# Expert kernel after linear attention: a second tile picked ahead, weight splits moved to GpSimd, attention's end and the first tiles reordered

## The chip, the cores and the metric

One Trainium2 chip, one core of it. The metric is the device time of one execution in microseconds (us). The engines are TensorE (PE, matmuls; PEld is its weight load), VectorE (DVE), ScalarE (ACT), GpSimd (POOL) and SyncE (SP), which in this kernel only issues DMAs.

## The reference

Three stages. First attention with a fading state, for 4 batches, 8 heads, 768 steps, 48 channels:

```
state = f[t] * state + k[t] (outer) v[t];   y[t] = q[t] @ state
```

Its output, 3072 tokens of 384 columns, goes to a layer of 8 experts. Each token takes the expert with the largest `x @ w_gate + bias[modality]`; `h = relu(x @ w1[e])` (1024 wide), `out = prob * (h @ w2[e])`. Last comes a gated layer on all tokens: a norm, `silu(xn @ w_gate) * (xn @ w_val)` (1536 wide), `@ w_out`. All in float32.

## The kernel before, in words

**Precision.** A float32 product is made from three matmuls: every operand is split in a rounded part (hi) and the rest (lo), and hi hi + lo hi + hi lo is summed (`three`, L1777). So each weight and each activation costs a rounding copy on ACT (hi) and a subtraction on DVE (lo).

**Attention** (`attention`, from L245) runs over CH = 6 chunks of 128 steps by B = 4 batches: 24 groups. The five engines each run a `step(c, b, half, more)` in a software pipeline; `tile(c, b, back)` gives the group that is `back` steps behind. In step n PE turns the keys of group n-1 (`ks_ps`), makes its scores, makes the output rows and gate logits of group n-3, and the state growth and the read (`yT_ps`) of group n-2. After the last chunk come four more steps with c = 6. Each finished chunk is routed on DVE: `Routing.choose` finds each token's expert, PE counts (`count`), `Routing.place` gives each token a row in its expert's region of `x_regions` in memory; GpSimd scatters the rows there (L137, four scatters per chunk). At c = 6 the chunk routed is the fifth. The sixth is chosen, counted, placed and scattered in the expert stage.

**Picked ahead.** `Ahead.pick` (L191 on) runs on DVE after four chunks: the expert with most tokens so far has a full tile of 256 tokens already, and SP loads its weights (`load_weights`) and rows (`load_rows`) while attention ends. ACT and DVE split w1 and x in the last four steps (`hi_w1`, `lo_w1`, `hi_x`, `lo_x`); w2 is split in the first tile.

**Barriers.** A block of engine programs ends with a barrier of all five engines. Then each reads a flag that says whether the fast attention was exact enough (`general_attention`, not run here), and a second barrier follows.

**Experts** (`experts`, from L1104). Tiles of 256 tokens of one expert, 13 of them here, in order j = 0 to 12 by `tiles` (L1263): `body(0, "first")`, a loop of `"middle"` ones, and `"last"`. On PE (`body` at L1801) a tile is: hidden(0), hidden(1), gather_y(0), hidden(2), gather_y(1), hidden(3), the turn of the next tile's x, gather_y(2), gather_y(3). hidden(g) is 18 matmuls into `h_ps`, gather_y(g) 12 into `y_ps`. In the first tile the count of the last chunk stands between hidden(0) and hidden(1) and waits for choose (`marks`, 7). gather_y(g) waits for `h_split` (DVE's lo_h, L1691) and `w2_split` (DVE's lo_w2, L1664).

ACT and DVE have their own written-out order for each place: hi_h(g) (L1484) and lo_h(g), next_w1(g) and next_w2(g) for the next tile's weights (L1457, L1461 and L1658, L1664), hi_x and lo_x. In the first tile DVE also computes `table_of_tiles` (which expert and which rows each tile has), `shifted_scores`, `rows_of_tiles`, and at its end `rows_of_tokens` and `gates_of_tokens`.

SP issues, in order, the loads of w1, x, w2 (one buffer each, so a piece is loaded when the piece of the tile before is split), the stores of y, a block of padding rows (`pad`), and the six thirds of the last stage's weights (`load_third`, into `g_in`), and its output weights at tile 7 (`WO_AT`). All of SP's loads for tile 1 wait for `table_ready`. ACT rounds thirds 0 and 1 in the first tile and one each at the end of tiles 1 to 4; GpSimd makes their lo part (L1419, three subtractions of 128x512 each) and, after each third, four scatters of gates (`by_token`, L1422).

The last stage (`body2`) is not touched but for the first square and the table load.

## Time and profile before

| | us |
|---|---|
| median of 3 runs | 866.95 (866.81 to 869.07) |
| the profiled execution | 866.84 |
| its span (first to last instruction) | 865.1 |
| TensorE busy in the span | 833.0 (96%), 5332 matmuls |
| DVE busy | 471.8 (55%), 773 instructions |
| ACT busy | 389.6 (45%) |
| GpSimd busy | 165.6 (19%) |
| mean granted TensorE clock | 0.988 |

The chain of work that ended last is 78% TensorE. Attention lies at 0 to 157.7, the experts at 160.3 to about 407, the gated layer behind them. In the page's list the clock is 9 or more tenths in nearly all of the 40 slices. Times in the rows are counted from the start of the span. `[3.17 <-issue]` at the end of a row means that the engine was idle for 3.17 us before this instruction, and what the profile names as releaser.

### The profile page before, as it was taken

What the parts mean: (1) busy time and instruction counts of PE and PEld (TensorE: products, weight loads), DVE (VectorE), ACT (ScalarE), POOL (GpSimd) and SP (SyncE); (2) the same over time, 40 slices, a digit from 0 to 9 for tenths busy, and PEclk for the clock granted to TensorE, in tenths of its full rate; (3) what the DMA queues carried; (4) which work ended last, traced back from release to release, by engine and by line L of the source; (5) the groups of instructions that cost most, each with busy time, mean ns of one, the idle gap of its engine ahead of it and who ended that gap; (6) DMA issues with size and microseconds to landing.
All of it is one profiled execution on the core that took longest, in us unless ns stands there. A gap on an engine that the chain in (4) does not pass through costs nothing.

```text
span 865.1 us, 15457 instructions
## 1 busy us (share of the span) xinstructions
PE 833.0 (96%) x5332; PEld 762.5 (88%) x5332; DVE 471.8 (55%) x773; ACT 389.6 (45%) x750; POOL 165.6 (19%) x165
## 2 busy tenths in 40 slices
PE   6999999779999999989999999999999999999997
PEld 6798988779999999989888888888888898888887
DVE  7989898687766666653444333334333333433332
ACT  5988786375666555653423411331241133123112
POOL 5444352318554000000000200100020010001001
PEclk9999999889999999999999999999999999999999
DMA  9877666497988797750200200100020000000000
GB/s 182 188 148 169 150 146 210 153 387 239 301 258 260 245 344 255 255 147 20 74 1 1 74 0 1 66 8 0 0 73 0 0 28 8 0 0 36 0 0 36
DMA packets 44082, 96.49 MB, mean 112 GB/s; under 512 B 9168, under 2 KB 25040, under 8 KB 43920
## 3 DMA queue, kind: packets, MB, share of 16 engines
q1 hardware_dynamic: 39952, 85.81, 33.6%
q0 software_dynamic: 3840, 9.47, 3.1%
q10 hardware_dynamic: 256, 0.79, 0.4%
q8 instruction: 18, 0.29, 0.1%
q14 instruction: 16, 0.13, 0.1%
HBM read 76.75 MB, written 19.29 MB: 111 GB/s over the span
## 4 chain that ended last, share of the span: by engine, by line
PE 78%; issue 2%; DVE 1%; POOL 0%; ACT 0%; DVEq 0%; ACTq 0%
PE h_ps L1779 16%; PE h_ps L1781 15%; PE h_ps L1780 15%; PE ym_ps L1779 7%; PE ym_ps L1781 7%; PE ym_ps L1780 7%; PE xTm_ps L1780 3%; PE xTm_ps L1779 3%; PE xTm_ps L1781 3%; PE xT_ps L1796 1%; PE xTm_ps L1787 1%; POOL out L1443 0%; DVE h_lo L1691 0%; DVE w_lo L1664 0%; ACT w_hi L1461 0%
## 5 line engine op out<-in xcount | busy, mean ns | idle before, releaser
L1754 DVE TENSOR_TENSOR gs<-h_ps,sig 128x512 f32<-128x512 f32 x72 | 49.8, 691 | 175.5 <-ACT sig L1555 175.5
L1555 ACT ACTIVATE sig<-h_ps 128x512 f32<-128x512 f32 x72 | 43.1, 598 | 158.9 <-PE h_ps L1781 158.9
L1566 ACT CAST h_hi<-hid 128x512 fp32r<-128x512 f32 x72 | 44.6, 620 | 150.2 <-DVE hid L1757 150.2
L1779 PE MATMUL h_ps<-x_hi,w_hi 128*128 128x256 f32 x312 | 89.7, 287 | 7.7 <-DVEq L1682 5.1
L1781 PE MATMUL h_ps<-x_lo,w_hi 128*128 128x256 f32 x312 | 89.3, 286 | 0.0
L1780 PE MATMUL h_ps<-x_hi,w_lo 128*128 128x256 f32 x312 | 89.1, 285 | 0.0
L1779 PE MATMUL h_ps<-w_hi,wg_hi 128*128 128x512 f32 x216 | 85.5, 396 | 0.0
L1781 PE MATMUL h_ps<-w_lo,wg_hi 128*128 128x512 f32 x216 | 84.6, 392 | 0.0
L1781 PE MATMUL h_ps<-w_lo,wv_hi 128*128 128x512 f32 x216 | 84.2, 390 | 0.0
L1780 PE MATMUL h_ps<-w_hi,wv_lo 128*128 128x512 f32 x216 | 84.0, 389 | 0.0
L1779 PE MATMUL h_ps<-w_hi,wv_hi 128*128 128x512 f32 x216 | 84.0, 389 | 0.0
L1780 PE MATMUL h_ps<-w_hi,wg_lo 128*128 128x512 f32 x216 | 83.9, 388 | 0.0
L1757 DVE TENSOR_TENSOR hid<-h_ps,gs 128x512 f32<-128x512 f32 x72 | 49.8, 692 | 57.5 <-PE h_ps L1781 57.5
L1779 PE MATMUL ym_ps<-w_hi,h_hi 128*128 128x384 f32 x208 | 73.0, 351 | 7.1 <-issue 3.5
L1664 DVE TENSOR_TENSOR w_lo<-w_in,w_hi 128x768 fp32r<-128x768 f32 x52 | 55.1, 1061 | 36.2 <-ACT w_hi L1461 36.1
L1767 DVE TENSOR_TENSOR h_lo<-hid,h_hi 128x512 fp32r<-128x512 f32 x72 | 49.8, 692 | 44.7 <-ACT h_hi L1566 44.7
L1781 PE MATMUL ym_ps<-w_lo,h_hi 128*128 128x384 f32 x208 | 71.2, 342 | 0.0
L1780 PE MATMUL ym_ps<-w_hi,h_lo 128*128 128x384 f32 x208 | 71.0, 342 | 0.0
L1779 PEld LDWEIGHTS h_ps<-x_hi,w_hi 128*128 128x128 f32 x312 | 60.7, 194 | 8.4 <-DVEq L1682 5.2
L1780 PEld LDWEIGHTS h_ps<-x_hi,w_lo 128*128 128x128 f32 x312 | 60.4, 194 | 0.0
L1781 PEld LDWEIGHTS h_ps<-x_lo,w_hi 128*128 128x128 f32 x312 | 60.4, 194 | 0.0
L1461 ACT CAST w_hi<-w_in 128x768 fp32r<-128x768 f32 x52 | 43.3, 835 | 34.2 <-PE ym_ps L1781 27.5
(222 smaller groups left out, 1890.0 us busy)
## 6 DMA issues: line engine op xcount, KB each, us to landing
w_raw<-in_w SPq DMA_DIRECT2D x52, 384.0 KB, 5.0
w_in<-in_w SPq DMA_DIRECT2D x52, 384.0 KB, 5.1
qkf_in<-in_qkf SPq DMA_DIRECT2D x43, 288.0 KB, 5.0
y_sorted<-x_group SPq DMA_DIRECT2D x13, 384.0 KB, 3.4
v_in<-in_v SPq DMA_DIRECT2D x24, 192.0 KB, 4.3
x_regions<-zero_row SPq DMA_DIRECT2D x12, 384.0 KB, 2.9
x_group<-x_regions SPq DMA_DIRECT2D x12, 384.0 KB, 3.9
g_in<-in_wg SPq DMA_DIRECT2D x3, 768.0 KB, 8.1
```

Of the source, the lines that this page charges most:

```text
L1461: nc.scalar.copy(w2_hi[:, 2 * g:2 * g + 2].rearrange("p b d -> p (b d)"), w2_in[:, g]).then_inc(w2_hi_done, 1)
L1555: nc.scalar.activation(sig[:], g_ps, ACT.Sigmoid).then_inc(sig_done, 1)
L1566: nc.scalar.copy(h2_hi[:, fb % HELD], hid[:]).then_inc(h2_hi_done, 1)
L1664: nc.vector.tensor_tensor(w2_lo[:, 2 * g:2 * g + 2].rearrange("p b d -> p (b d)"), w2_in[:, g], w2_hi[:, 2 * g:2 * g + 2].rearrange("p b d ...
L1754: nc.vector.tensor_tensor(gs[:], g_ps, sig[:], ALU.mult).then_inc(gs_done, 1)
L1757: nc.vector.tensor_tensor(hid[:], v_ps, gs[:], ALU.mult).then_inc(hid_done, 1)
L1767: nc.vector.tensor_tensor(h2_lo[:, fb % HELD], hid[:], h2_hi[:, fb % HELD].bitcast(F32), ALU.subtract).then_inc(h2_split, 1)
L1779: nc.tensor.matmul(out, hi, rhs_hi, start=first, stop=False)
L1780: nc.tensor.matmul(out, lo, rhs_hi, start=False, stop=False)
L1781: return nc.tensor.matmul(out, hi, rhs_lo, start=False, stop=last)
L1787: mm = nc.tensor.transpose(xT_ps[:, k, s * P:(s + 1) * P], x_in[:, s, k * P:(k + 1) * P], ident[:])
L1796: mm = nc.tensor.transpose(xT2_ps[:, k % 2, q * P:(q + 1) * P], y_in[par][:, q, k * P:(k + 1) * P], ident[:])
```

## The change

It has these parts.

1. **Attention's end.** The key turns and the copy `ks` of the last group are left out (nobody reads them). PE's read of a group is now a function `read`, and that of the last group goes into `ks_ps` right after the one before it, ahead of the output rows of group 22. ACT's order of rounding copies changes; the split of w1's fourth piece on DVE (`lo_w1(3)`) moves behind the barriers. SP issues the eight weight loads ahead of the last two v loads.
2. **A second pick.** `pick_next`, 12 small DVE instructions at the start of the expert stage, finds the expert with most tokens left after five chunks and the row from which its tile starts. SP loads tile 1's weights and x from it at once, and not from the table. `table_of_tiles` and `rows_of_tokens` allow for two tiles out of order.
3. **w2 of the first tile.** ACT rounds all four pieces before hi_h(0), GpSimd subtracts (four times 128x768), ahead of the last chunk's scatters, and signals on `made`.
4. **New order in the first tiles.** DVE: pick_next, choose, lo_w1(3), lo_h(0), place, lo_h(1), table, and so on. `rows_of_tiles` goes to the first tile's end, `shifted_scores`, `rows_of_tokens` and `gates_of_tokens` to the ends of tiles 1, 2 and 3. The thirds are rounded at the ends of tiles 1 to 6, the gates' scatters stand behind thirds 3 to 5 (eight each), output weights are loaded at tile 8. The exp is in tile 2.
5. **Last tile.** ACT takes hi_h(0) before the squares, and loads its table of functions there.

```diff
@@ class Ahead
+    def pick_next(self, nc, rt, link, ready):
+        link(nc.vector.tensor_tensor(self.has[:], rt.base[:], self.start[:], ALU.subtract))
+        link(nc.vector.tensor_reduce(self.most[:], self.has[:], AX.X, ALU.max))
+        link(nc.vector.tensor_scalar(self.has[:], self.has[:], self.most[:, 0:1], None, ALU.is_equal))
+        link(nc.vector.tensor_tensor(self.has[:], self.has[:], rt.rank_e[:], ALU.mult))
+        link(nc.vector.tensor_reduce(self.next_rank[:], self.has[:], AX.X, ALU.max))
+        nc.vector.tensor_scalar(self.next_f[:], self.next_rank[:], -1.0, float(E), ALU.mult, ALU.add)
+        nc.vector.tensor_scalar(self.next_expert[:], self.next_rank[:], -1.0, float(E), ALU.mult, ALU.add)
+        link(nc.vector.tensor_scalar(self.next_one[:], rt.rank_e[:], self.next_rank[:, 0:1], None, ALU.is_equal))
+        link(nc.vector.tensor_tensor(self.next_at[:], self.next_one[:], self.start[:], ALU.mult))
+        nc.vector.scalar_tensor_tensor(self.start[:], self.next_one[:], float(TM), self.start[:], ALU.mult, ALU.add)
+        link(nc.vector.tensor_reduce(self.next_row_f[:], self.next_at[:], AX.X, ALU.add))
+        nc.vector.tensor_scalar(self.next_row[:], self.next_row_f[:], 1.0, None, ALU.add).then_inc(ready, 1)
@@ attention, sync
-            for b in range(2):
-                load_v(*tile(CH, b, 2))
             sp.wait_ge(ahead_sems.picked, PICKS)
             e = first.expert_of(sp)
             first.load_weights(sp, e, w1, w2, ahead_sems)
+            for b in range(2):
+                load_v(*tile(CH, b, 2))
@@ attention, scalar
+                if at(c, CH) and b == 1:
+                    first.hi_w1(nc, act, 3, ahead_sems)
+                    kept(tile(c, b, 2), ks_ps)
...
-                if at(c, CH) and b < 2:
-                    first.hi_w1(nc, act, 2 * b, ahead_sems)
...
                 if at(c, CH) and b == 0:
-                    first.hi_w1(nc, act, 1, ahead_sems)
+                    for g in range(2):
+                        first.hi_w1(nc, act, g, ahead_sems)
+                if (t := tile(c, b, 2)) and not (at(c, CH) and b == 1):
+                    kept(t, yT_ps)
+                if at(c, CH) and b == 0:
+                    first.hi_w1(nc, act, 2, ahead_sems)
@@ attention, vector
-                if at(c, CH) and b == 2:
+                if at(c, CH) and b == 1:
+                    first.lo_w1(nc, dve, 2, ahead_sems)
                     dve.wait_ge(flag_sum, 1)
...
+                if at(c, CH) and b == 2:
+                    first.lo_x(nc, dve, xT_ps, ahead_sems)
                 if t := tile(c, b, 3):
...
-                if at(c, CH) and b == 2:
-                    first.lo_x(nc, dve, xT_ps, ahead_sems)
-                    first.lo_w1(nc, dve, 3, ahead_sems)
@@ attention, tensor
                     pe.wait_ge(scaled, n + 1)
-                    wait_past(pe, ks_done, n)
-                    for j in range(PR):
-                        mm = nc.tensor.transpose(ks_ps[:, j], kT[:, s, j], ident[:])
-                    mm.then_inc(k_turned, 1)
+                    if not at(c, CH):
+                        wait_past(pe, ks_done, n)
+                        for j in range(PR):
+                            mm = nc.tensor.transpose(ks_ps[:, j], kT[:, s, j], ident[:])
+                        mm.then_inc(k_turned, 1)
...
+                if at(c, CH) and b == 1:
+                    pe.wait_ge(ks_done, NT - 1)
+                    read(c, b, tile(c, b, 2), ks_ps)
+                    pe.wait_ge(small_ready, 1)
+                    nc.tensor.matmul(flag_ps, rt.ones_r[:], small[:], start=True, stop=True).then_inc(flag_sum, 1)
                 if t := tile(c, b, 3):
@@ experts, sync
-            for i in range(EARLY):
-                load_third(i)
-            sp.dma_start(norm.g_norm[:], rms_g).then_inc(norm_in, 16)
...
                 if place == "first":
                     sp.wait_ge(table_ready, 1)
-                    e1 = expert(1)
-                    pad(e1)
+                    e1 = sp.value_load(first.next_expert[0:1, 0:1], min_val=0, max_val=E - 1)
+                    row = sp.value_load(first.next_row[0:1, 0:1], min_val=0, max_val=E * REGION - TM)
                     for g in range(GR):
                         sp.wait_ge(w1_split, g + 1)
                         load_w1(e1, g)
+                    sp.dma_start(x_in, x_regions[bass.ds(row, TM), :].rearrange("(s p) d -> p s d", p=P)).then_inc(x_landed, 16)
+                    for g in range(GR):
+                        sp.wait_ge(made, MADE + g + 1)
+                        load_w2(e1, g)
+                    for i in range(EARLY + 1):
+                        load_third(i)
                     sp.wait_ge(scattered, 16 * B)
-                    load_x(1)
-                    for g in range(GR):
-                        sp.wait_ge(w2_split, g + 1)
-                        load_w2(e1, g)
-                    load_third(EARLY)
-                    sp.wait_ge(rows_ready, 1)
+                    sp.wait_ge(table_ready, 2)
@@ experts, gpsimd
+            for g in range(GR):
+                pool.wait_ge(w2_hi_done, g + 1)
+                nc.gpsimd.tensor_tensor(w2_lo[:, 2 * g:2 * g + 2].rearrange("p b d -> p (b d)"), w2_in[:, g],
+                                        w2_hi[:, 2 * g:2 * g + 2].rearrange("p b d -> p (b d)").bitcast(F32), ALU.subtract
+                                        ).then_inc(made, 1)
             pool.wait_ge(marks, Routing.PLACED)
@@ experts, scalar
-            hi_w2(0, 0)
+            for g in range(GR):
+                hi_w2(0, g)
...
+                hi_h(0)
+                if place != "first":
+                    next_w1(0)
                 if place == "last":
                     act.wait_ge(norm_in, 16)
                     square(0, 0)
-                hi_h(0)
+                hi_h(1)
+                if place == "last":
+                    nc.scalar.preload_act_table_set("sigmoid_and_others")
@@ experts, vector
+            first.pick_next(nc, rt, link, table_ready)
             rt.choose(nc, dve, CH - 1, marks, 0)
-            lo_w2(0, 0)
-            dve.wait_ge(counted, 1)
-            rt.place(nc, dve, CH - 1, LAST_HALF, pre_ps, cnt_ps, marks, 0)
+            lo_w1(0, GR - 1)
...
                 lo_h(0)
                 if place == "first":
-                    table_of_tiles()
+                    dve.wait_ge(counted, 1)
+                    rt.place(nc, dve, CH - 1, LAST_HALF, pre_ps, cnt_ps, marks, 0)
...
                 lo_h(1)
+                if place == "first":
+                    table_of_tiles()
...
                 if place == "first":
-                    rows_of_tokens()
-                    gates_of_tokens()
+                    rows_of_tiles()
+                if place == "middle":
+                    with dve.If(j < 4):
+                        with only(dve, j, 1):
+                            shifted_scores()
+                        with only(dve, j, 2):
+                            rows_of_tokens()
+                        with only(dve, j, 3):
+                            gates_of_tokens()
@@ experts, tensor
-                    pe.wait_ge(w2_split, j * GR + g + 1)
+                    if place == "first":
+                        pe.wait_ge(made, MADE + g + 1)
+                    else:
+                        pe.wait_ge(w2_split, j * GR + g + 1)
```

## Rows read from the trace of the kernel before

**Rows 1.** Busy time per stretch: length, engines busy (instructions), TensorE clock, DMA share, GB/s.
```profile
155.30:160.30 5.00, 0.00 (x1) 0.03 (x1) 2.04 (x4) 1.19 (x2) 0.79 (x5) 0.81 0.18 66
...
160.30:184.80 24.50, 22.42 (x130) 21.79 (x130) 19.12 (x58) 13.96 (x19) 4.40 (x7) 0.83 0.78 279
...
184.80:209.20 24.40, 19.74 (x127) 19.23 (x127) 19.40 (x29) 12.21 (x18) 16.07 (x13) 0.93 0.89 316
...
209.20:226.90 17.70, 17.70 (x128) 17.68 (x127) 14.12 (x14) 11.56 (x16) 11.33 (x9) 1.00 0.87 275
...
192.50:196.20 3.70, 3.65 (x12) 3.68 (x13) 2.80 (x3) 0.00 (x0) 3.70 (x3) 0.54 1.00 386
...
178.90:182.60 3.70, 3.70 (x16) 3.61 (x16) 3.52 (x6) 2.62 (x4) 0.00 (x0) 0.55 1.05 413
```

**Rows 2.** Timeline of TensorE: start, length; in brackets the idle time before.
```profile
160.30 0.55 PE L1779 MATMUL h_ps<-x_hi,w_hi 128*128 128x256 f32 x1 [5.06 <-DVEq L1682]
...
178.28 0.44 PE L1779 MATMUL ym_ps<-w_hi,h_hi 128*128 128x384 f32 x1 [1.83 <-DVE h_lo L1691]
...
192.55 0.66 PE L1779 MATMUL ym_ps<-w_hi,h_hi 128*128 128x384 f32 x1 [3.17 <-issue]
...
207.05 0.44 PE L1779 MATMUL ym_ps<-w_hi,h_hi 128*128 128x384 f32 x1 [1.49 <-DVE h_lo L1691]
...
393.43 0.42 PE L1779 MATMUL ym_ps<-w_hi,h_hi 128*128 128x384 f32 x1 [0.32 <-issue]
```

**Rows 3.** Attention's end: last scatter, DVE's last subtraction, GpSimd's last wait.
```profile
154.80 0.97 POOL L137 DMA_INDIRECT x_regions<-x_group,row  x1 [0.30 <-issue]
...
156.76 0.95 DVE L226 TENSOR_TENSOR w_lo<-w_raw,w_hi 128x768 fp32r<-128x768 f32 x1
...
L516 POOLq EVENT_SEMAPHORE  x1: 43/43/43, 157.4 to 157.4; - x1
```

**Rows 4.** Timeline: DVE's bookkeeping and its place in an ordinary tile.
```profile
172.51 0.36 DVE L1623 TENSOR_TENSOR scratch<-scratch,most_all 128x192 f32<-128x192 f32 x1
...
187.56 0.16 DVE L1636 SCALAR_TENSOR_TENSOR moved_up<-one_expert,tokens_before 128x8 f32<-128x8 f32 x1
...
190.04 0.18 DVE L1648 TENSOR_SCALAR pos<-pos_f 128x24 uint32<-128x24 f32 x1
...
190.72 0.30 DVE L1654 RECIPROCAL of_token<-total 128x24 f32<-128x24 f32 x1
...
191.76 0.69 DVE L1691 SCALAR_TENSOR_TENSOR h_lo<-h_ps,h_hi 128x512 fp32r<-128x512 f32 x1 [0.73 <-issue]
...
228.40 0.96 DVE L1664 TENSOR_TENSOR w_lo<-w_in,w_hi 128x768 fp32r<-128x768 f32 x1 [1.50 <-ACT w_hi L1461]
...
231.28 0.34 PE L1779 MATMUL ym_ps<-w_hi,h_hi 128*128 128x384 f32 x1
```

**Rows 5.** Timeline: DVE and GpSimd (POOL) side by side, three places.
```profile
201.56 4.84 DVE L1664 TENSOR_TENSOR w_lo<-w_in,w_hi 128x768 fp32r<-128x768 f32 x1 [0.64 <-ACT w_hi L1461]
...
201.78 3.79 POOL L1419 TENSOR_TENSOR wg_lo<-g_in,wg_hi 128x512 fp32r<-128x512 f32 x3
...
229.83 5.24 POOL L1419 TENSOR_TENSOR wv_lo<-g_in,wv_hi 128x512 fp32r<-128x512 f32 x3 [7.89 <-ACT wv_hi L1453]
...
232.83 1.09 DVE L1658 TENSOR_TENSOR w_lo<-w_raw,w_hi 128x768 fp32r<-128x768 f32 x1
...
128.94 0.73 DVE L204 TENSOR_SCALAR one_expert<-rank_e,has_rank 128x8 f32<-128x8 f32 x1
...
128.64 1.06 POOL L137 DMA_INDIRECT x_regions<-x_group,row  x1 [8.69 <-DVE row L132]
```

**Rows 6.** Timeline: first and seventh step of choose, ACT's rounding of output weights.
```profile
160.18 0.19 DVE L100 TENSOR_TENSOR biased<-logits,token_bias 128x32 f32<-128x32 f32 x1 [2.47 <-PEq L796]
...
161.56 0.23 DVE L109 TENSOR_TENSOR_SCAN upto<-restart,chosen 128x32 f32<-128x32 f32 x1
...
162.28 0.83 ACT L1461 CAST w_hi<-w_in 128x768 fp32r<-128x768 f32 x1 [5.79 <-SPq L1337]
```

More of the change, by code:

```diff
@@ L544, in step @@
                         neg_logs(*t)
-                if t := tile(c, b, 1):
+                if (t := tile(c, b, 1)) and not at(c, CH):
                     _, s, n = t
@@ L722, in growth, with read @@
                 mm.then_inc(ds_done, 1)
+            def read(c, b, t, acc):
+                cc, s, n = t
+                if not tile(c, b, 1):
+                    pe.wait_ge(masked, n + 1)
+                if at(c, 0):
+                    pe.wait_ge(consts, CONSTS)
+                pe.wait_ge(v_landed[s], (cc + 1) * 16)
+                if not at(c, CH) and not (at(c, 0) and b == 2):
+                    growth(s, n)
+                wait_past(pe, state_done, n - 3)
+                if not at(cc, 0):
+                    for j in range(PR):
+                        nc.tensor.matmul(acc[:, j], state[:, s, j], qT[:, s, j], start=(j == 0), stop=False,
+                                         skip_group_check=True)
+                if at(cc, 0):
+                    pe.wait_ge(yT_zero, 1)
+                for j in range(PR):
+                    for par in range(2):
+                        h, r = 2 * j + par, PAD * par
+                        mm = nc.tensor.matmul(acc[r:r + D, j], v_in[:, s, D * h:D * (h + 1)],
+                                              scores[:, s % 2, par, j], start=at(cc, 0), stop=(at(cc, 0) or j == PR - 1),
+                                              skip_group_check=True)
+                mm.then_inc(y_done, 1)
             def step(c, b, half, more):
@@ L782, in step @@
                 if at(c, CH) and b == 1:
-                    pe.wait_ge(small_ready, 1)
-                    nc.tensor.matmul(flag_ps, rt.ones_r[:], small[:], start=True, stop=True).then_inc(flag_sum, 1)
                     first.turn(nc, pe, xT_ps, ident, ahead_sems)
```

163 lines of the change are left out of this document (70 added, 93 removed).

## The prediction

> **What bounds the kernel now.** I read the stage table first. The ordinary expert tile (209.2 to 226.9) is 17.7 us long and the matmul unit is busy for all of it, at full clock, so nothing that the change does to an ordinary tile can shorten it. Tile 0 takes 24.5 us and tile 1 takes 24.4, with 22.4 and 19.7 us of busy time, and the clock was 0.83 and 0.93 in them [rows 1]. So there are some 13.5 us above the ordinary length in those two tiles, and 5.0 us more in which the matmul unit does nothing between attention and tile 0. That is all the change can win.
>
> The timeline of TensorE then shows where they lie [rows 2]: 5.06 us before the first expert matmul, 1.83 us before group 2's output matmuls of tile 0, 3.17 us in tile 1 before its first output matmul, 1.49 us later in tile 1, 0.32 us in the last tile. After 1.83 and after 3.17 us of idleness the granted clock fell from 2.4 to about 1.2 GHz for a stretch (0.55 and 0.54 over 3.7 us [rows 1]); in 3.7 us at 0.54 the unit does 2.0 us of full-speed work, so each such stretch costs 1.7 us. After 1.49 us it didn't fall.
>
> The DVE, GpSimd and queue rows say who is late. At the end of attention GpSimd waits until 157.4 for its last row scatter to land, and DVE's last subtraction ends at 157.7 [rows 3]; the barrier follows them at once, and then the flag is read by all five engines, 2.3 us that stay. In tile 1 the 3.17 us are DVE's: it works through the rows and gates of the tokens from 187.56 to 191.0 and comes to h_lo only at 191.76 [rows 4]. The 1.49 us come from a DVE subtraction that took 4.84 us instead of 0.96 while GpSimd ran three subtractions of its own [rows 5].
>
> **The change, part by part.** The sum is made against the profiled execution, 866.84 us (span 865.1), 0.11 under the median of the runs.
>
> *Attention's end.* Group 23's key transposes and their copy go (their state is never used), its scores come 0.6 us earlier, and its read goes into the freed buffer, so it needn't wait for the copy of group 22. DVE loses one 768-column subtraction ahead of the barrier (it moves behind it) and does the x subtraction sooner: its end comes some 2.6 us earlier. GpSimd's four scatters however start when DVE has placed the fifth chunk's tokens, which moves by 0.6 us only, and their landing then is at 156.8. The barrier was at 157.7, so the gain is **-0.9** (bounds: -0.5 if the scatters don't move with it, -2.6 if they land early enough not to matter). On SP, the eight weight loads pass two v loads that waited; v is wanted at 147 and lands by about 141, so this is nothing either way.
>
> *Tile 0, DVE.* Ahead of the body DVE now runs pick_next (12 small instructions), then choose, then one 0.96 us subtraction. The matmul unit counts the chosen tokens between hidden(0) and hidden(1), and for that waits for choose. Choose's first and seventh instruction started 1.38 us apart, 0.23 for each with its wait [rows 6]; its whole chain is 1.7, and pick_next at the same price, with some that don't wait, 2.4. Without interference choose ends 4.1 us after DVE starts, at about 163.3, when hidden(0) at half clock also ends: a wait of 0 to 0.8.
>
> *Tile 0, GpSimd.* The four subtractions of the output weights go from DVE to GpSimd, where 128x512 takes 1.26 (three in 3.79 [rows 5]), so 128x768 about 1.9, four of them 7.6 us. ACT's rounding (0.83 each [rows 6]) feeds them from 160.0, so they fill 160.1 to about 168. gather_y(0) to (3) want them at 166, 171, 175 and 178 at the earliest: ready in time. That takes away the 0.25 and 1.83 us stalls and the slow stretch behind them, **-3.9**. But the same 8 us hold all of choose. Two rows show what DVE does beside a subtracting GpSimd: with both operands in SBUF it waited 3.9 us, through all three GpSimd instructions; in another tile it waited 0.13 us for the one running and went first at the next boundary [rows 5]. A DVE instruction on 8 columns took 0.73 us while GpSimd issued a scatter [rows 5], so small ones wait as well. I take one wait per GpSimd subtraction, the milder row: after seven instructions of pick_next (until 160.5) four waits are due (the one-hot compare, the row product, the start update, choose's first sum), the last of them ends at about 167.6, and the other six steps of choose end at 169.1. The wait of the matmul unit is then 169.1 - 163.3 = **+5.8**, and hidden(1) runs part of its 18 matmuls at 1.2 GHz, +1.0; the earlier start of the tile and its count give 0.7 back. Tile 0: -3.9 + 5.8 + 0.3 = **+2.2**, ending at 186.1 instead of 184.8. Lower bound: no waits, -4.7; upper: held through the whole run, +3.3.
>
> The Trainium skill, page "SBUF — State Buffer", section "Who interferes with whom", has a rule that speaks against this part: a DVE instruction with two SBUF inputs and a GpSimd instruction that reads SBUF share one read port, and whichever comes second is blocked until the first has ended. By that rule alone the 0 waits are ruled out and the sum is the forecast's; the row of 4.84 us is worse than the rule, as there DVE lost three turns in a row.
>
> *Tile 1's inputs.* Picked ahead, its weights are loaded from about 168 even in the blocked case, and x behind them; they are wanted from 173 on. ACT and DVE have its splits done before tile 0 ends. The scatters of the last group land at about 179 and hold up only SP's loads for tile 2, wanted at 187 and later. Cost 0. The early loads of g_in move behind them; their first use is now at the end of tile 1.
>
> *DVE's bookkeeping moves.* At tile 0's end only rows_of_tiles is left (1.3 us) in place of 3.5: with 0.7 us of loop entry DVE reaches h_lo about 1.0 us late, so 3.17 becomes 1.0, the slow stretch (1.7) goes, and so does the 1.49, since GpSimd has no subtractions in tile 1: 1.0 - 3.17 - 1.7 - 1.49 = **-5.4**.
>
> In an ordinary tile DVE's last weight subtraction frees it at 229.27, and h_lo, 0.69 long, has to be done by 231.28 [rows 4]: 1.3 us are free. shifted_scores (three of about 0.36 [rows 4], 1.1 in a chain) fits at the end of tile 1, or waits once for the first piece of the g_in subtraction that GpSimd starts at that moment: **+0.3** (0 to 0.7). rows_of_tokens at the end of tile 2 doesn't fit. It had 11 instructions in 2.6 us (187.56 to 190.13) and has 20, the added ones mostly on 1 to 24 columns: 3.8 us. With some 0.5 of loop h_lo starts at 2.3 + 3.8 + 0.5 = 6.6 after the tile's end and ends at 7.4 instead of 4.3: a stall of 3.1. GpSimd runs its three subtractions over the same time; about half of the DVE instructions from there on read two SBUF tensors, and it would be 5.5 if it waited for each of the three. I take **+3.7**, and with a stall of over 3 us a slow stretch, **+1.7** (0 to 1.7). gates_of_tokens at tile 3's end is 1.0: it fits.
>
> *Last tile.* ACT rounds h before it squares, so the 0.32 us go: **-0.3**. The table load, 1.3 us, moves there from tile 0; ACT waits for matmuls for 4 us next, which covers it.
>
> Sum: -0.9 + 2.2 - 5.4 + 0.3 + 3.7 + 1.7 - 0.3 = +1.3, so **868.1 us**. The measurement can tell about 0.3%, 2.6 us, from no change.
>
> **Rivals.** *Small DVE instructions slip between* GpSimd's subtractions in tile 0, and choose ends at 163.3 to 164. Tile 0 then is -4.7 in place of +2.2, and the total 866.84 + 1.3 - 6.9 = **861.2** (858.5 with no slow stretch and a bare 3.1 us stall in tile 3, 863.0 with 5.5). For it: no row shows a small two-tensor DVE instruction beside a subtracting GpSimd, and one of 0.2 us leaves the port soon. Against: the waits of [rows 5].
>
> *DVE is held through whole runs of GpSimd subtractions*, as in the row of 4.84. It decides from the point at which DVE's request comes in the middle of a GpSimd instruction that has others right behind it. Choose ends 1.1 later; shifted_scores waits until 3.3 us after its place, +2.6 over my term; rows_of_tokens +1.8: 868.1 + 5.5 = **873.6**, slower.
>
> *The change doesn't do what it says*: the second pick has under 256 tokens and a 14th tile appears, +17.6. The inputs' counts (about 1000 tokens left for the expert picked) are against it: 1 in 100.
>
> **How the numbers follow.** Forecast 0.45, own range 865 to 871 (the terms' bounds without tile 0's), rival one 0.37, rival two 0.14, the rest on either side 0.04. Of the forecast's 0.45 about 0.06 is faster by over 2.6, 0.24 within, 0.15 slower. Faster: 0.37 x 0.97 + 0.06 = 0.42; same: 0.24 + 0.02 = 0.26; slower: 0.32. The range of 8 in 10 runs from 859.0 to 872.5.
>
> **What would show it.** A gap of TensorE behind hidden(0) of tile 0, and DVE instructions on 8 to 32 columns of 1 us and more beside GpSimd's w_lo: forecast, over 5 us; rival one, under 1. No gap before gather_y(2) of tile 0. Under 1.2 us before tile 1's first output matmul. A gap of 3 to 6 us before tile 3's. If that last gap isn't there, my count of DVE's free time is wrong, and the whole forecast with it.

## The result and the profile after

The changed kernel takes 888.15 us (median of 4 runs, 885.16 to 888.68), the kernel before 868.01 (4 runs, 866.81 to 873.08). The ratio is 1.0214, 95% interval 1.0165 to 1.0262: slower by 2.1%, outside the range of 859.0 to 872.5. The profiled execution took 887.66 us, its span is 885.9, the granted clock 0.976 (before: 865.1 and 0.988).

The timeline of TensorE in the changed kernel, with the idle time in brackets as in [rows 2]:

```profile
161.23 0.55 PE L1823 MATMUL h_ps<-x_hi,w_hi 128*128 128x256 f32 x1 [5.67 <-DVEq L1729]
...
170.61 0.60 PE L117 MATMUL xTm_ps<-upto,before 128*128 128x8 f32 x2 [5.20 <-DVE upto L109]
...
195.26 0.41 PE L1823 MATMUL ym_ps<-w_hi,h_hi 128*128 128x384 f32 x1 [1.12 <-issue]
...
213.95 0.41 PE L1823 MATMUL ym_ps<-w_hi,h_hi 128*128 128x384 f32 x1 [0.71 <-issue]
...
237.54 0.66 PE L1823 MATMUL ym_ps<-w_hi,h_hi 128*128 128x384 f32 x1 [5.61 <-issue]
...
295.95 0.41 PE L1823 MATMUL ym_ps<-w_hi,h_hi 128*128 128x384 f32 x1 [2.19 <-issue]
...
311.04 0.44 PE L1823 MATMUL ym_ps<-w_hi,h_hi 128*128 128x384 f32 x1 [2.02 <-issue]
```

The 1.83, 3.17 and 1.49 us of [rows 2] are gone; 5.20 in tile 0, 1.12 in tile 1 and 5.61 in tile 3 are the gaps that the prediction named. The two at 295.95 and 311.04 it did not. Gone too are the gap before gather_y(2) of tile 0 and the 0.32 us of the last tile. So all four signs that the prediction named came true, and the time was still 20 us off: they looked at tiles 0 to 3 only.

The same by stretches, cut at the turns of x, with two short ones behind tile 0's gap at the end (columns as in [rows 1]):

```profile
161.20:186.80 25.60, 20.37 (x113) 20.07 (x114) 20.92 (x57) 8.92 (x13) 11.55 (x12) 0.69 0.68 249
186.80:203.90 17.10, 15.98 (x116) 15.65 (x115) 11.43 (x20) 9.39 (x14) 0.00 (x0) 1.00 0.87 320
203.90:222.60 18.70, 17.99 (x129) 17.81 (x128) 13.92 (x16) 11.56 (x16) 4.62 (x3) 1.00 0.75 246
222.60:248.10 25.50, 19.89 (x129) 19.71 (x128) 16.95 (x33) 11.81 (x17) 3.74 (x3) 0.87 0.73 226
248.10:265.80 17.70, 17.70 (x128) 17.70 (x127) 12.60 (x16) 11.57 (x16) 5.27 (x3) 1.00 0.73 222
...
283.60:306.10 22.50, 19.87 (x128) 19.35 (x127) 10.66 (x12) 10.58 (x16) 15.09 (x13) 0.92 0.76 209
306.10:326.20 20.10, 18.08 (x129) 17.74 (x128) 13.08 (x14) 12.24 (x17) 13.22 (x10) 1.00 0.66 199
326.20:344.60 18.40, 17.99 (x129) 17.81 (x128) 11.12 (x13) 10.20 (x15) 5.50 (x6) 1.00 0.99 289
...
170.60:175.00 4.40, 4.39 (x20) 4.39 (x21) 2.46 (x10) 0.00 (x0) 1.28 (x2) 0.50 0.98 374
170.60:177.00 6.40, 6.39 (x27) 6.39 (x28) 3.12 (x12) 1.29 (x2) 2.94 (x3) 0.50 1.02 357
```

With the starts of the turns (L1831 here, L1787 before) the two traces are laid side by side. A stretch from one turn to the next is called by the tile whose turn ends it. From the first expert matmul to the turn in tile 0: 25.56 us against 21.52. Then 17.08 against 20.84 (tile 1), 18.69 against 19.48 (tile 2), 25.50 against 17.64 (tile 3), 17.75 and 17.74 (tiles 4 and 5), and 22.54, 20.10, 18.39 (tiles 6, 7 and 8), all against 17.64; every one after them is 17.74 against 17.64. The texts written ahead of the experiments call the three late stretches tiles 5 to 7. From the last turn to the end it is 488.1 us against 484.2. So of the 20.8 us of span, 0.9 lie ahead of the first expert matmul, -0.5 in the three stretches to tile 2's turn, +7.9 in tile 3's, +8.1 in the three of tiles 6 to 8, 0.5 in the ordinary tiles, 3.9 behind the last turn.

DVE and GpSimd in tile 0, where the prediction put its four waits:

```profile
162.27 0.15 DVE L222 TENSOR_SCALAR next_f<-next_rank 128x1 f32<-128x1 f32 x1
...
162.40 1.44 DVE L224 TENSOR_SCALAR next_one<-rank_e,next_rank 128x8 f32<-128x8 f32 x1
163.87 1.74 DVE L225 TENSOR_TENSOR next_at<-next_one,start_behind 128x8 f32<-128x8 f32 x1
165.64 1.72 DVE L226 SCALAR_TENSOR_TENSOR start_behind<-next_one,start_behind 128x8 f32<-128x8 f32 x1
...
167.54 1.61 DVE L100 TENSOR_TENSOR biased<-logits,token_bias 128x32 f32<-128x32 f32 x1
...
170.33 0.23 DVE L109 TENSOR_TENSOR_SCAN upto<-restart,chosen 128x32 f32<-128x32 f32 x1
...
161.97 1.84 POOL L1446 TENSOR_TENSOR w_lo<-w_in,w_hi 128x768 fp32r<-128x768 f32 x1 [0.26 <-ACT w_hi L1506]
```

Each of the four long ones (L224, L225, L226, L100) waits for one GpSimd subtraction, and none for two. The instruction on one column at 162.27 did not wait, though GpSimd's subtraction had begun at 161.97. In tile 3, DVE's rows of the tokens and GpSimd's three subtractions:

```profile
230.96 0.69 DVE L1683 TENSOR_SCALAR in_first<-row_all,first_row 128x24 f32<-128x24 f32 x1
231.56 1.31 DVE L1684 TENSOR_SCALAR in_next<-row_all,next_row_at 128x24 f32<-128x24 f32 x1
232.91 1.19 DVE L1685 SCALAR_TENSOR_TENSOR in_first<-row_all,first_end,in_first 128x24 f32<-128x24 f32 x1
...
230.32 3.74 POOL L1461 TENSOR_TENSOR wg_lo<-g_in,wg_hi 128x512 fp32r<-128x512 f32 x3 [13.97 <-ACT wg_hi L1498]
```

Again one wait for each GpSimd instruction: in experiment 4, where GpSimd is held back, the same three took 0.24, 0.23 and 0.24, which is 2.5 us less. The next question is what lies behind the rest: tile 3's 7.9 instead of 5.4, the 8.1, and the 0.10 us by which all tiles are longer.

### The profile page after: what moved, and what is told of

It reads as the page before. It is cut to its first block, busy times and chain, and to the rows that moved or that the text cites. A ratio compares the mean times of both kernels' runs of the same rounds, so it can differ in the third digit from the quotient of the medians.

```text
span 885.9 us, 15519 instructions
## 1 busy us (share of the span) xinstructions
PE 841.9 (95%) x5328; PEld 770.2 (87%) x5328; DVE 474.8 (54%) x792; ACT 388.4 (44%) x749; POOL 172.5 (19%) x169
## 4 chain that ended last, share of the span: by engine, by line
PE 78%; issue 2%; DVE 1%; POOL 0%; ACT 0%; DVEq 0%; ACTq 0%
PE h_ps L1825 15%; PE h_ps L1824 15%; PE h_ps L1823 15%; PE ym_ps L1823 7%; PE ym_ps L1825 7%; PE ym_ps L1824 7%; PE xTm_ps L1825 3%; PE xTm_ps L1823 3%; PE xTm_ps L1824 3%; PE xTm_ps L1831 1%; PE xT_ps L1840 1%; POOL out L1488 0%; DVE next_at L225 0%; DVE start_behind L226 0%; DVE biased L100 0%
## 5 line engine op out<-in xcount | busy, mean ns | idle before, releaser
L1710 DVE TENSOR_TENSOR w_lo<-w_in,w_hi 128x768 fp32r<-128x768 f32 x48 | 47.6, 991 | 41.6 <-ACT w_hi L1506 37.0
L1825 PEld LDWEIGHTS h_ps<-x_lo,w_hi 128*128 128x128 f32 x312 | 62.2, 199 | 0.8 <-issue 0.8
L1824 PEld LDWEIGHTS h_ps<-x_hi,w_lo 128*128 128x128 f32 x312 | 62.2, 199 | 0.0
```

What stands on the lines that cost most here:

```text
L1710: nc.vector.tensor_tensor(w2_lo[:, 2 * g:2 * g + 2].rearrange("p b d -> p (b d)"), w2_in[:, g], w2_hi[:, 2 * g:2 * g + 2].rearrange("p b d ...
L1824: nc.tensor.matmul(out, lo, rhs_hi, start=False, stop=False)
L1825: return nc.tensor.matmul(out, hi, rhs_lo, start=False, stop=last)
```

## The experiments

They ran in four groups, each on one chip: 1 to 4 on chip A, 5 to 8 on chip B, 9 to 12 on chip C, 13 to 16 on chip A again. Each group has its own runs of the kernel before; times are medians, ratios are to the kernel before of the same group, with their 95% interval.

**1. The changed kernel again** (no edit).

> The changed kernel itself, unaltered, as the reference of the runs that follow. Between the profiles of the two kernels lie 20.8 us of span; tile by tile the turns of x show +4.9 by tile 0, back to +0.4 by tile 2, +8.3 by tile 3, +13.4 by tile 6, +15.9 by tile 7, +16.6 by tile 8, and a further +4.2 in work that both kernels do alike (ordinary tiles 17.74 against 17.64 us, the last stage 466.1 against 462.9). If the last 4.2 and the 1.5 us by which attention began later belong to that execution and not to the change, this run is 1 to 5 us shorter than 887.66 and its ordinary tile is 17.64 to 17.70. If they belong to the change, it is 887 to 889 again with 17.74. Either way the stalls of tile 0 (5.2), tile 3 (5.6) and tiles 5 to 7 are there again.

888.11 us against 869.51, ratio 1.022 (1.0189 to 1.025). The stretches are 25.21, 17.09, 18.69, 25.32, 17.76, 17.74, 22.36, 19.25, 18.21, then 17.74; 488.1 behind the last turn. So nearly everything is the kernel's. Two things are not steady: in the profiles of the experiments, two aside, the first expert matmul starts anywhere from 158.6 to 164.4, and tile 7's stretch is 20.10, 19.25 and, in experiment 13, 23.73 with the same program.

**2. Fewer gate scatters in a row.**
```diff
-                for n in range(max(i - KD, 0) * (NT // KD), max(i - KD + 1, 0) * (NT // KD)):
+                for n in range([0, 0, 0, 0, 4, 8, 12][i], [0, 0, 0, 0, 4, 8, 12][i + 1]):
...
+            for turn, lo, hi in [(9, 12, 16), (11, 16, 20), (12, 20, 24)]:
+                pool.wait_ge(x_split, turn)
+                for n in range(lo, hi):
...
```


> The 24 small scatters of the gates go out four at a time (tiles 4 to 7, 9, 10) instead of eight at a time in tiles 4, 5 and 6; the thirds and their loads stay where they are. Theory (scatters): eight in a row take half of the load rate for 10 us, and the expert's weights then come too late; the stretches between the turns of x, 22.5, 20.1 and 18.4 us in the tiles after 283, go back to about 17.7, and the time falls by 7 to 9 us against the changed kernel. Rival (thirds): what makes those tiles late is the load, rounding and splitting of a third of 768 KB in each, now in tiles 4 to 6, and the scatters are only beside it: the stretches stay above 20 and 18.5 us and the time changes by less than 2 us.

881.78 us, 6.3 below experiment 1, a little less than the 7 to 9 expected; experiment 1's three stretches were 6.6 us too long. Here they are 17.74, 17.83 and 18.17, no gap of TensorE over 0.3 us is left in them. On chip A the bunches of eight make those tiles late, not the thirds. (The third and fourth bunch ran one right behind the other, from 317.4 to 330.0, beside the 18.17.)

**3. The choice ahead of GpSimd's subtractions.**
```diff
+            pool.wait_ge(marks, Routing.CHOSEN)
             for g in range(GR):
                 pool.wait_ge(w2_hi_done, g + 1)
```


> GpSimd waits for DVE's choice of the last tokens before its four subtractions of tile 0's output weights; nothing else is altered. Theory (port): DVE's instructions of 1.44 to 1.74 us fall back to under 0.3, the choice ends about 5 us earlier, TensorE's 5.2 us behind hidden(0) go to under 0.8, the output weights' low halves are ready at about 165.5, 167.5, 169.5 and 171.5 and hold up the first output matmul by at most 0.5: the time falls by 4 to 5.5 us. Rival (chain): pick_next and the choice are 19 dependent steps and late by themselves, then the gap stays above 3 us, and the later weights add to it: the time changes by less than 1.5 us or grows.

883.98 us, 4.1 below experiment 1. The 5.2 us gap is gone and tile 0's stretch is 18.81 instead of 25.21, as the port theory has it, but the next one is 19.95 instead of 17.09: TensorE waits 1.90 us for DVE's h_lo. The waits have moved on to the placing of the tokens, in DVE's rows of this kernel:

```profile
169.63 0.51 DVE L129 TENSOR_TENSOR rows<-upto,shift 128x32 f32<-128x32 f32 x1
170.17 1.78 DVE L130 TENSOR_TENSOR rows<-rows,chosen 128x32 f32<-128x32 f32 x1
171.98 0.21 DVE L131 TENSOR_REDUCE row_f<-rows 128x4 f32<-128x32 f32 x1
172.22 1.51 DVE L132 CAST row<-row_f 128x4 uint32<-128x4 f32 x1
173.65 1.88 DVE L133 COPY row_all<-row_f 128x4 f32<-128x4 f32 x1
```

A cast and a copy of four columns, with one SBUF input each, wait as long as the multiplication. The Trainium skill (page "SBUF — State Buffer", section "Who interferes with whom") says that copy, cast and tensor_scalar can take the pair of ports shared with GpSimd if their operands meet certain conditions, and that tensor_reduce never does on this chip. The rows agree: the reduction between them took 0.21, and the tensor_scalar on one column at 162.27 in the changed kernel 0.15.

**4. The second third behind the tokens' rows.**
```diff
                 pool.wait_ge(g_hi_done, i + 1)
+                if i == 1:
+                    pool.wait_ge(pos_ready, 1)
```


> GpSimd's subtraction of the second third (tile 2's end) waits until DVE has placed the tokens' rows. Theory one (too many DVE instructions): the gap of TensorE in tile 3 falls only by the waits of the four long ones (0.69, 1.31, 1.19 us against 0.2 each), from 5.6 to about 3.2, and stays over 2.5 us; the slow stretch may go or stay: -2.4, or -4 with it. Theory two (the port alone): the gap goes to under 1 us and the time falls by 6.5 to 8 us.

883.09 us, 5.0 below. The gap is 3.13 us instead of 5.61, and the stretch 22.42 instead of 25.32: theory one, 20 instructions don't fit, and GpSimd adds 2.5 to that. The stretch explains 2.9 of the 5.0; the rest is within the spread of four runs each (881.48 to 885.1 here).

**5. 32 bytes of padding** ahead of the expert weights.
```diff
+        self.pad = sb("pad", [P, 8])
         self.w1_raw = sb("w1_raw", [P, 2, QB, DM])
```


> One unused SBUF tile of 32 bytes a partition, ahead of the expert weights; no instruction is altered. In every profile of the changed kernel an ordinary tile is 17.74 us, in that of the kernel before 17.64, and the output matmuls run at 0.1770 us each instead of 0.1737 while the hidden ones keep 0.120; the seven new small tiles have moved all weight tiles from addresses that divide by 64 to ones that leave 32. Theory (address): the matmul unit reads 384-column operands a little slower from such addresses: the ordinary tile goes back to 17.64 us and the last stage is about 3 us shorter, together 4 to 5 us off the changed kernel. Rival (chip or order): the 0.1 us are the chip's or come from the engines' order: 17.74 stays and the time stays within 1 us.

879.59 us; ratio 1.0125 (1.011 to 1.0139). The theory fell: the ordinary tile is still 17.73 us, 488.0 behind the last turn. But the stretches of tiles 6 to 8, with eight scatters in a row, are 17.73, 17.83, 17.73 here.

**6. Attention's end alone**, on the kernel before (the hunks of the diff within attention, and the fourth w1 subtraction behind the choice).
```diff
             rt.choose(nc, dve, CH - 1, marks, 0)
+            lo_w1(0, GR - 1)
             lo_w2(0, 0)
```


> The kernel before with attention's end alone changed (group 23's key transposes and copy left out, its read in the freed buffer, the new order of the first expert's splits, weights loaded ahead of the last v tiles, the fourth w1 subtraction behind the barrier). Prediction on record: -0.9 us. From the two profiles: the stretch from DVE's masking of group 22's scores to the first expert matmul was 18.22 us and is 17.60, thus -0.6; the first expert matmul moves by that and the fourth subtraction adds to DVE's work in tile 0, so -0.6 to +0.4 in all, same within 0.3%. Rival: the new order costs attention time elsewhere, as the first matmul came 0.9 us later in the changed kernel: +0.9 to +2. The ordinary tile is 17.64 us here if the address or the change of the tiles makes the 0.1 us, 17.74 if the chip does.

Ratio 0.9991 (0.9975 to 1.0007): -0.8 us, with an interval of 1.4 to either side. From the masking of group 22's scores (144.32) to the first expert matmul (161.94) it is 17.62 us against 18.22, so 0.6 less where 0.9 was forecast. The ordinary tile is 17.64 on the chip where experiment 5 had 17.73: the 0.1 us is the change's.

**7. rows_of_tokens in two pieces**, ahead of the tile's last subtraction.
```diff
                 next_w2(2)
-                next_w2(3)
-                if place == "first":
-                    rows_of_tiles()
                 if place == "middle":
                     with dve.If(j < 4):
...
                         with only(dve, j, 3):
-                            gates_of_tokens()
+                            places_of_tokens()
+                next_w2(3)
...
```


> The changed kernel with DVE's rows_of_tokens cut in two, the first 14 instructions in tile 2 and the last 6 in tile 3, and with these and shifted_scores put ahead of the last subtraction of the tile's output weights, where DVE otherwise waits 1.5 us for ScalarE; the gates stay at tile 3's end. Theory (DVE has no room for 20 instructions behind its last subtraction, GpSimd's subtractions make it worse): the gap of 5.6 us in tile 3 goes to under 0.7, the slow stretch with it, tile 3's stretch from 25.3 to 17.8: the time falls by 7 to 8 us. Rival (only moved): the pieces push the last subtraction and h_lo back, and stalls of 1 us and more appear in tiles 1, 2 and 3: the time falls by less than 4 us.

870.76 us; ratio 1.0021 (1.0006 to 1.0036). The stretches of tiles 2, 3 and 4 are 17.74, 17.86 and 17.92, and the gap of 0.71 at the boundary 1 to 2 has gone with the 5.61. Against experiment 5 on the same chip it is 8.8 us. This kernel has no padding, and the stretches of tiles 6 to 8 are 17.74, 17.74 and 17.83: it was not the padding that made them short in experiment 5.

**8. Everything so far together**, with DVE's h(3) of tile 0 ahead of two weight subtractions.
```diff
+                if place == "first":
+                    lo_h(3)
                 next_w1(2)
                 next_w2(1)
-                lo_h(3)
+                if place != "first":
+                    lo_h(3)
```


> Everything together: scatters four at a time, GpSimd's output-weight subtractions behind the choice, rows_of_tokens in two pieces, the 32-byte tile, and in tile 0 DVE's subtraction of h(3) ahead of two weight subtractions (it came 1.9 us late with the choice first). Theory (the causes are separate and add up): -6.5 for the scatters, -5.5 for tile 0 and its follower, -7.5 for tile 3, -4.3 for the address, thus 24 us below the changed kernel, 864 to 866, and 3 to 5 us below the kernel before on the same chip. Rival (they share their time: a tile that starts earlier only waits for the same late loads): less than 18 us, 870 or more.

868.32 us, ratio 1.0003 (0.9989 to 1.0017), above the 864 to 866 expected and below the rival's 870. From the first expert matmul to the last turn it is 216.3 us against 220.6 before, so 4.3 are won in the tiles, and 3.8 more behind the last turn take them back. The padding did nothing for the address loss, and tile 1 lost 0.76, 0.97 and 1.32 us.

**9. The old addresses**: the thirteen new SBUF tiles allocated behind all others.
```diff
-        self.next_rank = sb("next_rank", [P, 1])
...
         h_lo = sb("h_lo", [P, HELD, 2, TM], F32R)
+        first.next_rank = sb("next_rank", [P, 1])
```


> The changed kernel with its thirteen new small SBUF tiles set behind all others, so that every tile that the kernel before has lies at the address it had there; no instruction is altered. So far: the 32-byte tile, which only brought the addresses back to a multiple of 64, left the ordinary tile at 17.73 and the stretch from the last turn of x to the end at 488 us, against 17.64 and 484.2 in the kernel before and in the one with attention's end alone. Theory (addresses, in a wider pattern than 64): 17.64 and 484.2 return, 4 to 5 us off. Rival (the program's instructions): 17.74 and 488 stay. The 9 us of tiles 5 to 7: if they are there or not is chance of the layout, so -9 or 0 beside the above.

873.56 us, ratio 1.0084 (1.0054 to 1.0113). The ordinary tile is 17.64 and 483.6 us lie behind the last turn, with not one instruction altered. The stretches of tiles 6 to 8 are 17.64, 17.72, 17.64.

```profile
352.66 0.82 PE L1831 MATMUL xTm_ps<-ident,x_group 128*128 128x128 f32 x6
370.30 0.82 PE L1831 MATMUL xTm_ps<-ident,x_group 128*128 128x128 f32 x6
```

**10. The kernel before, all shifted by 224 bytes.**
```diff
+        self.pad = sb("pad", [P, 56])
         self.w1_raw = sb("w1_raw", [P, 2, QB, DM])
```


> The kernel before with one unused SBUF tile of 224 bytes a partition ahead of the expert weights, so that these and all tiles behind them lie 224 bytes further, the output weights and h by the same amount. Theory one (a tile's own address matters): ordinary tile 17.74, the stretch after the last turn 487 to 488, the time +4 to +5 us. Theory two (the distance between the output weights and h matters, which the change made 320 bytes longer and this kernel leaves alone): 17.64 and 484, the time unchanged. Rival (instructions): also 17.64 and unchanged.

869.4 us; ratio 1.0005 (0.9979 to 1.003), at most 2.6 us where theory one has 4 to 5. Its profiled execution took 1427.73 us at a granted clock of 0.666, so the tile's length at full clock isn't known.

**11. The kernel before with bunches of eight.**
```diff
-                for n in range(i * (NT // 6), (i + 1) * (NT // 6)):
+                for n in range(max(i - KD, 0) * (NT // KD), max(i - KD + 1, 0) * (NT // KD)):
```


> The kernel before with the gates' 24 small scatters in three bunches of eight behind the fourth, fifth and sixth third, where it had six bunches of four; the thirds stay in their tiles. Theory (eight in a row are too much for the loads): tiles with a bunch are late by 1 us and more, +2 to +10 us in all. Rival (it takes the third's load in the same tile and the changed layout too): the loads of the thirds come two tiles earlier here, the tiles stay at 17.64, and the time is unchanged.

866.88 us, ratio 0.9993 (0.9973 to 1.0012); all tiles from 2 on at 17.64. This is on chip C; no run puts bunches of eight into the kernel before on chip A.

**12. Kernel 5 with bunches of twelve.**
```diff
-                for n in range(max(i - KD, 0) * (NT // KD), max(i - KD + 1, 0) * (NT // KD)):
+                for n in range([0, 0, 0, 0, 0, 12][i], [0, 0, 0, 0, 12, 24][i]):
```


> The kernel with the 32-byte tile, which had no late tile with eight scatters in a row, with the 24 scatters in two bunches of twelve (tiles 5 and 6). Theory (the scatters fill the time in which the weights must land, and eight are at the edge): with twelve the stall is back, at least 2 us in tile 6 or 7, +3 to +12 us against the 879.6 of that kernel. Rival (the number doesn't matter, the layout alone decides): all tiles at 17.7 to 17.9, 879 to 880 again.

878.15 us, stretches of 17.7 to 17.8. On chip C even twelve in a row make nothing late. The number of scatters alone can't be the answer, and the chip had changed between the groups.

**13 and 14. Kernels 1 and 9 again, side by side on chip A.**

> The changed kernel once more, unaltered, on the chip of e14 to e16. Theory one (the chip): the late tiles 5 to 7 belong to the two chips seen first; here they are at 17.74 and 17.83 and the time is 878 to 881. Theory two (the layout): they belong to this kernel's layout in SBUF; they are late again (22.4, 19 to 23, 18.2) and the time is 885 to 890 while e14 beside it has none.

> The changed kernel with every old tile at its old address, as in e9, beside e13 on one chip. Against e13: -5 us if only the 0.1 us a tile and 3.8 us behind the last turn are the layout's (theory one of e13), -14 us if the late tiles are too (theory two).

It was chip A again, so neither theory was tested as it was meant, and still it is settled, since kernel 14 is kernel 9. 13: 889.57 us, the three stretches 22.51, 23.73 and 18.34. 14: 884.06, 5.5 less, ordinary tile 17.64, and the three stretches 22.53, 20.02 and 18.33, where the same program had 17.64, 17.72 and 17.64 on chip C. First kernel 14 on chip A, its transfers from 5.5 to 9 us behind the turn in tile 5 (the DMA view of that window; q1 carries the loads, q0 the scatters):

```profile
DMA packets 125, 0.24 MB, mean 70 GB/s; under 512 B 46, under 2 KB 46, under 8 KB 125
...
q1 hardware_dynamic: 88, 0.24, 53.5%
q0 software_dynamic: 37, 0.00, 0.7%
```
Then kernel 9 on chip C, the same 3.5 us:
```profile
DMA packets 423, 0.92 MB, mean 262 GB/s; under 512 B 126, under 2 KB 126, under 8 KB 423
...
q1 hardware_dynamic: 332, 0.91, 96.3%
q0 software_dynamic: 91, 0.00, 1.9%
```
The loads are late, but so is work that waits for no load. ScalarE in kernel 14, whose turn in tile 5 began at 284.46:
```profile
286.02 0.60 ACT L1530 ACTIVATE h_hi<-h_ps 128x512 fp32r<-128x512 f32 x1 [2.69 <-PE h_ps L1825]
287.49 0.80 ACT L1510 CAST x_hi<-xTm_ps 128x768 fp32r<-128x768 f32 x1 [0.86 <-remote]
...
291.86 0.83 ACT L1506 CAST w_hi<-w_in 128x768 fp32r<-128x768 f32 x1 [2.84 <-remote]
```
and in kernel 9, whose turn began at 282.02:
```profile
282.22 0.60 ACT L1530 ACTIVATE h_hi<-h_ps 128x512 fp32r<-128x512 f32 x1 [1.33 <-PE h_ps L1825]
282.87 0.80 ACT L1510 CAST x_hi<-xTm_ps 128x768 fp32r<-128x768 f32 x1
...
284.95 0.83 ACT L1506 CAST w_hi<-w_in 128x768 fp32r<-128x768 f32 x1 [0.55 <-PE ym_ps L1825]
```
ScalarE starts h_hi 1.56 us behind the turn instead of 0.20, though TensorE had done the same work at the same point; in the kernel this instruction waits for TensorE's h alone. Whether the signal came late or ScalarE took it up late, the trace doesn't show.

**15. The kernel before with 320 bytes ahead of h alone.**
```diff
+        pad = sb("pad", [P, 80])
         h_hi = sb("h_hi", [P, HELD, 2, TM], F32R)
```


> The kernel before with one unused SBUF tile of 320 bytes a partition ahead of h_hi, so that the weights stay and h's two parts lie 320 bytes further, which is the distance that the change gave them. Theory (the distance between the output weights and h decides how fast TensorE runs the output matmuls): ordinary tile 17.74, 488 us behind the last turn of x, the time +4.5 to +5.5 us. Rival (something else in the order of the tiles): 17.64, 484.2, unchanged.

872.44 us; the ratio of 1.0019 (0.9989 to 1.0048) can't tell by itself, the trace can: all ten stretches from tile 2 on are 17.73 or 17.74, and 487.2 us lie behind the last turn. In all traces at full clock, the end is 483.6 to 485.2 us with h at its old distance from the weights and 487.2 to 489.4 with 320 bytes more.

```profile
353.39 0.82 PE L1788 MATMUL xTm_ps<-ident,x_group 128*128 128x128 f32 x6
371.12 0.82 PE L1788 MATMUL xTm_ps<-ident,x_group 128*128 128x128 f32 x6
388.86 0.82 PE L1788 MATMUL xTm_ps<-ident,x_group 128*128 128x128 f32 x6
```

**16. All causes undone.** Kernels 2, 7 and 9, h(3) as in 8, and GpSimd's order in tile 0:
```diff
+            pool.wait_ge(marks, Routing.CHOSEN)
             for g in range(GR):
+                if g == 2:
+                    pool.wait_ge(marks, Routing.PLACED)
+                    for b in range(B):
+                        rt.scatter(nc, LAST_HALF, b, x_regions).then_inc(scattered, 16)
                 pool.wait_ge(w2_hi_done, g + 1)
```


> Old addresses; GpSimd: two of the output-weight subtractions behind DVE's choice, then the four row scatters, then the other two; DVE's h(3) of tile 0 ahead of two weight subtractions; rows_of_tokens in two pieces ahead of the last subtraction; the gates' scatters four at a time. The combination of e8 was at 868.3 us, as the kernel before, with 4.9 us of address loss in it, 0.76 and 0.97 us of stalls in tile 1 and 1.32 before tile 2's first turn of x, whose rows landed late. Theory (sums of separate causes): 862 to 864, 0.4 to 0.7% below the kernel before; if the earlier scatters don't bring x in time, 864 to 865. Rival (DVE and GpSimd only wait for each other in another place of tile 0): 866 or more.

864.95 us against 869.18, ratio 0.9961 (0.9938 to 0.9985): 0.4% faster than the kernel before, at the upper edge of what was expected, on the chip on which the changed kernel loses 2.2%. In its profile 217.4 us lie between the first expert matmul and the last turn (220.6 before). What it still loses:

```profile
182.55 0.44 PE L1839 MATMUL ym_ps<-w_hi,h_hi 128*128 128x384 f32 x1 [1.88 <-DVE h_lo L1747]
...
190.56 0.41 PE L1839 MATMUL ym_ps<-w_hi,h_hi 128*128 128x384 f32 x1 [0.75 <-issue]
...
200.38 0.88 PE L1847 MATMUL xTm_ps<-ident,x_group 128*128 128x128 f32 x6 [0.96 <-DMA x_group<-x_regions]
...
246.25 0.41 PE L1839 MATMUL ym_ps<-w_hi,h_hi 128*128 128x384 f32 x1 [1.11 <-issue]
...
243.55 1.31 DVE L1709 TENSOR_SCALAR total<-total 128x24 f32<-128x24 f32 x1
...
243.52 3.78 POOL L1463 TENSOR_TENSOR wg_lo<-g_in,wg_hi 128x512 fp32r<-128x512 f32 x3 [12.25 <-ACT wg_hi L1506]
```

The last of these gaps lies beside DVE's gates_of_tokens, one instruction of which waited for a GpSimd subtraction once more. The stretches of tiles 8 and 11, each beside a bunch of scatters, are 18.19.

## Why the prediction was wrong

In short, of the 19.5 us between the forecast 868.1 and the profiled 887.66, two terms of the sum that were too small make 4.7 (the slow matmuls behind tile 0's gap, and tile 3's stall), and things for which the sum had no term make most of the rest: the late tiles 6 to 8 (8.1) and longer output matmuls in every tile and in the last stage (about 5).

**Attention's end, forecast -0.9.** -0.6 by the trace of experiment 6, -0.8 by its times, whose interval includes zero. Right in sign and size as far as it can be told.

**Tile 0, forecast +2.2.** The mechanism was right to the instruction, the gap 5.20 instead of 5.8. Up to tile 0's turn it cost 4.0 us (25.56 against 21.52). The term that was too small is "hidden(1) runs part of its 18 matmuls at 1.2 GHz, +1.0": behind the gap the clock was 0.50 for the whole 6.4 us to 177.0, in which full speed needs 3.2, so +3.2. The chosen value, one wait per GpSimd instruction, held; rival one (no waits) and rival two (held through the run) are both out. Removing the waits gains 6.4 us in that stretch, of which 2.9 come back in the next (experiment 3).

**Tile 1 and the boundary, forecast -5.4 and +0.3.** The gap was 1.12 us against 1.0, that at the boundary 0.71 against 0.3. The two stretches gave -3.8 and -0.8. With tile 0, -0.5 instead of -2.9: the missing 2.4 are 2.2 of tile 0's clock, 0.4 of the boundary, 0.1 of tile 1's gap and 0.3 of the longer ordinary tile, less the 0.6 by which tile 0's gap was shorter.

**Tile 3, forecast +3.7 and +1.7.** 7.9. The step that failed is the size: I worked out 3.1 us for the 20 instructions alone and 5.5 with one wait for each of GpSimd's three, and took 3.7, between them. Experiment 4 measured the first at 3.13 and the changed kernel the second at 5.61. Tile 0 was priced at one wait per GpSimd instruction and tile 3 at less, for no reason that a row gave. The slow stretch was there both times (22.42 - 17.74 - 3.13 = 1.6, and 7.8 - 5.6 = 2.2).

**Last tile, forecast -0.3.** The gap of 0.32 us is gone.

**What had no term.** First, tiles 6 to 8, +8.1: the sum has nothing for any tile between tile 3 and the last, and the gates' scatters, which the change puts into bunches of eight, were counted nowhere. On chip A the three stretches are 6.6 to 11.9 us too long in the six traces with bunches of eight (the first profile among them); with the bunches of four of the kernel before (experiment 15) they are not, and with those of experiments 2 and 16 by 0.5 and 0.6. On chips B and C eight and twelve cost nothing. The chip of the changed kernel's first profile isn't recorded, but its stretches are those of chip A. Second, about 5 us for 13 small SBUF tiles (0.1 in each expert tile, the rest behind the last turn; experiment 14 is 5.5 below 13): the sum took every matmul to last as long as before. Third, at 887.66 the execution began its tiles 0.9 us late where 0.6 less was due, by chance.

So the sum of the named parts would have been -0.6 - 0.5 + 7.9 - 0.3 = +6.5, about 873, slower. The late tiles and what the layout costs outside the stretches above (0.5 in the ordinary tiles, 4.2 at the end) bring it to 886, the late start to 887.7. On chip B the changed kernel with its 32 bytes took 879.59, 1.25% over the kernel before. It would have been outside the range there too.

**Still open.** Why chip A delays loads and engines beside eight small scatters in a row, and whether it is scatters alone or only together with the loads of the changed kernel. Its traces also lack many of the records by which a load's landing is known (w_raw's has no landing time in them), so what came first, a load or a signal, can't be read. Three chips were seen, and only one of them shows the late tiles. Which property of the distance between h and the output weights counts wasn't tried beyond 320 bytes, nor whether another tile than the output weights is its partner; h's own address moved too, and only experiment 10 argues for the distance, by its time alone.

## What to carry to other kernels

Price a wait in two places by the same rule: a chain of small DVE instructions beside a run of GpSimd subtractions waited once for each of them in tile 0, in tile 3 and in experiment 3, and a copy and a cast with one SBUF input waited as well as two-input ones. Ask of every part that is moved, and not only of the tiles that one looks at, what runs beside it in its new place. Allocate new small tiles behind the large ones (experiment 9), and compare the length of an undisturbed stage between two kernels before looking for the cause of a difference in the disturbed ones. And run the unchanged reference on the same chip in every group: a cost that appears on one chip and not on another looks exactly like the effect of whatever edit was made between the two.

## What the hardware showed unexpectedly

- The place of h in SBUF changes the matmul's rate. Mean distance of output matmuls of the last stage from one to the next: 0.174 us before, 0.177 in the changed kernel, whose h lies 320 bytes further from the weights; the first layer's matmuls of the expert tiles are at 0.12 in both. Over 13 tiles and the last stage this is about 5 us, 0.5%.
- Chips differ in what small scatters do to other work: the same program lost 7.9 us in three tiles (22.53 + 20.02 + 18.33 against 17.64 + 17.72 + 17.64) on chip A and none of it on chip C, while the kernel before had medians of 867.7 to 869.5 on all of them.
- DVE's waits for GpSimd also strike a cast and a copy of 128x4 (1.51 and 1.88 us), not a reduction of 128x32 (0.21) nor a tensor_scalar of 128x1 (0.15); one of 128x24 waited in experiment 16 (1.31).
